# Two sequence passes, one mean and one buffer of a three-stage kernel are moved across the seam between its first two stages

## What is computed

```
X   = fft(fft(x, axis=1), axis=2).real          # a spectrum: [2, 3008, 256]
xn  = x / sqrt(mean(x*x) + 1e-6) * rms_g        # per token
h   = silu(xn @ w_gate) * (xn @ w_val)          # up to 1536
x2  = h @ w_out                                 # down to 256
h2  = x2 @ w_in                                 # up to 2048
out = (h2 * cos(h2)) @ w_out2                   # down to 256
```

## Time and profile before

| what | value |
|---|---|
| median of three runs | 984.6 us |
| the profiled execution | 984.3 us |
| its span, first to last instruction | 982.5 us |
| TensorE busy | 972.3 us, 99% of the span |
| VectorE busy | 742.9 us |
| ScalarE busy | 638.7 us |
| GpSimd busy | 350.4 us |
| granted TensorE clock | full in all of 40 slices |

### The profile page before, as it was taken

One profiled execution on the slowest core, in us unless ns is written; L12 is line 12 of the kernel. 1 busy time (PEld: TensorE's weight loads), 2 busy tenths in 40 slices (PEclk: granted clock), 3 DMA queues, 4 the chain that ended last, 5 costly groups with the idle time before them and its releaser, 6 DMA issues.

```text
span 982.5 us, 13009 instructions
## 1 busy us (share of the span) xinstructions
PE 972.3 (99%) x4518; PEld 807.9 (82%) x4518; DVE 742.9 (76%) x1028; ACT 638.7 (65%) x803; POOL 350.4 (36%) x292
## 2 busy tenths in 40 slices
PE   8999999999999999999999999999999999999998
PEld 8978788888888888888888888888888888888886
DVE  6887987768876768877667877767887767887665
ACT  5586778764468774458775448776448776437777
POOL 0377874027730007750007751005661004770000
PEclk9999999999999999999999999999999999999999
DMA  9788002001010001010001010001000000000001
GB/s 332 235 221 235 1 1 53 0 1 43 1 43 1 1 0 42 0 40 2 0 0 42 0 32 11 0 0 42 0 32 0 0 0 7 36 0 0 0 0 42
DMA packets 14082, 36.80 MB, mean 37 GB/s; under 512 B 2618, under 2 KB 6682, under 8 KB 13658
## 3 DMA queue, kind: packets, MB, share of 16 engines
q1 hardware_dynamic: 11978, 31.63, 9.4%
q0 software_dynamic: 2064, 4.72, 2.7%
HBM read 22.35 MB, written 9.26 MB: 32 GB/s over the span
## 4 chain that ended last, share of the span: by engine, by line
PE 91%; DMA 3%; POOL 2%; DVE 2%; issue 1%; ACT 1%; SPq 0%; DVEq 0%; ACTq 0%; POOLq 0%
PE ps L541 30%; PE ps L543 30%; PE ps L542 30%; DMA x_sb<-x 1%; POOL work L1184 1%; PE ps L492 1%; DMA stat<-mean_row 1%; DMA w_lo<-w_f 1%; PE ps L510 1%; PE ps L508 0%; SPq L319 0%; POOL squares L1122 0%; POOL uv_t L1141 0%; POOL w_lo L1104 0%; POOL h_lo L1095 0%
## 5 line engine op out<-in xcount | busy, mean ns | idle before, releaser
L541 PE MATMUL ps<-h_hi,wo_hi 128*128 128x502 f32 x672 | 261.5, 389 | 0.6 <-DVE h_lo L980 0.6
L543 PE MATMUL ps<-h_hi,wo_lo 128*128 128x502 f32 x672 | 261.3, 389 | 0.0
L542 PE MATMUL ps<-h_lo,wo_hi 128*128 128x502 f32 x672 | 261.1, 389 | 0.0
L1095 POOL TENSOR_TENSOR h_lo<-work,h_hi 128x502 fp32r<-128x502 f32 x92 | 101.5, 1111 | 373.8 <-ACT h_hi L782 369.9
L767 ACT ACTIVATE h_hi<-work 128x502 fp32r<-128x502 f32 x132 | 82.4, 626 | 174.2 <-POOL work L1184 173.9
L1082 DVE SCALAR_TENSOR_TENSOR work<-work,ps 128x1004 f32<-128x1004 f32 (+1 forms) x109 | 117.2, 1075 | 95.6 <-ACT work L864 95.2
L1068 DVE SCALAR_TENSOR_TENSOR work<-work,ps 128x1004 f32<-128x1004 f32 (+1 forms) x109 | 116.5, 1074 | 48.0 <-ACT work L850 47.9
L541 PE MATMUL ps<-x_hi,win_hi 128*128 128x502 f32 x384 | 150.0, 391 | 0.0
L541 PEld LDWEIGHTS ps<-h_hi,wo_hi 128*128 128x128 f32 x672 | 126.2, 188 | 28.2 <-issue 0.8
L542 PE MATMUL ps<-x_lo,win_hi 128*128 128x502 f32 x384 | 149.3, 389 | 0.0
L543 PE MATMUL ps<-x_hi,win_lo 128*128 128x502 f32 x384 | 149.2, 389 | 0.0
(11 more groups left out here) (89 smaller groups left out, 1275.7 us busy)
## 6 DMA issues: line engine op xcount, KB each, us to landing
out<-y_sb SPq DMA_DIRECT2D x10, 502.0 KB, 3.0
x_sb<-x SPq DMA_DIRECT2D x6, 768.0 KB, 10.3
w_lo<-w_f POOLq DMA_DIRECT2D x6, 512.0 KB, 7.0
uv_t<-uv_dram SPq DMA_DIRECT2D x6, 502.0 KB, 3.5
wo_raw<-wo SPq DMA_DIRECT2D x1, 2048.0 KB, 8.5
win_raw<-win SPq DMA_DIRECT2D x1, 2048.0 KB, 9.4
raw_b<-w1b SPq DMA_DIRECT2D x3, 512.0 KB, 12.4
raw_a<-w1a SPq DMA_DIRECT2D x3, 512.0 KB, 12.3
```

Of the source, the lines that this page charges most:

```text
L541: nc.tensor.matmul(acc, w_hi, v_hi, start=start, stop=False)
L542: nc.tensor.matmul(acc, w_hi, v_lo, start=False, stop=False)
L543: return nc.tensor.matmul(acc, w_lo, v_hi, start=False, stop=stop)
L1095: nc.gpsimd.tensor_tensor(dst, src, hi.bitcast(F32), ALU.subtract).then_inc(s, 1)
```

## The change

Four things are changed. (1) The last group of three columns becomes one of two and one of a single column; in both DVE takes the second half and its turn, and the turns count on a semaphore of their own, `n1_turned`. (2) `plus[1]` moves out of `pq` to an address 1024 bytes into `x2_hi`, a buffer that is written and read only in the second half of a tile, when `plus` is not in use. (3) `sequence(32)` and `sequence(33)` move behind item 1's two up products and the eighth mean, which itself moves behind the second half of item 1; on ACT the last `uv_copy` and `mean_copy(7)` stand behind item 0's silu, ahead of `square(8)`; the seventh mean is taken at step 33 and not at step 32. (4) `w1_add(2)` is issued two places sooner on GpSimd.

```diff
-        plus = [sb(f"plus{i}", [N], o_pq + i * TB // 2) for i in range(2)]
+        plus = [sb("plus0", [N], o_pq), sb("plus1", [N], o_x2 + 1024)]
...
-        GROUPS = [range(i, i + 3) for i in range(0, H // 2, 3)]
+        GROUPS = [range(i, i + 3) for i in range(0, H // 2 - 3, 3)] + [range(H // 2 - 3, H // 2 - 1), range(H // 2 - 1, H // 2)]
...
-            return (1, 0) if g == NG - 1 else (0, 1)
+            return (1, 0) if g >= NG - 2 else (0, 1)
...
-        RMS_AT = [8, 9, 15, 20, 24, 28, 32]
+        RMS_AT = [8, 9, 15, 20, 24, 28, 33]
...
-            pe.wait_ge(n1_out, 3 * NG)
+            pe.wait_ge(n1_out, 3 * NG - 4)
+            pe.wait_ge(n1_turned, 4)
...
                 up1(t, 1, halves=(0,))
-                if first:
-                    rms(RMS_LATE[0])
-                else:
+                if not first:
                     down(t - 1, ITEMS - 1, tokens=(0,))
                 up1(t, 1, halves=(1,))
                 if not first:
                     down(t - 1, ITEMS - 1, tokens=(1,))
+                if first:
+                    rms(RMS_LATE[0])
+                    sequence(LAST - 2)
+                    sequence(LAST - 1)
...
             up1(0, 0, halves=(0,))
-            sequence(LAST - 2)
-            sequence(LAST - 1)
+            pe.wait_ge(pq_out, LAST)
             pe.wait_ge(mean_out, len(RMS_AT))
...
-                for c in range(1 if g == NG - 1 else 2):
+                for c in range(1 if g >= NG - 2 else 2):
...
-            for p in range(LAST // 2):
+            for p in range(LAST // 2 - 1):
...
                     if first and i == 0:
+                        uv_copy(LAST // 2 - 1)
+                        mean_copy(RMS_LATE[0])
                         square(MEANS - 1)
-                        mean_copy(RMS_LATE[0])
...
-            dve.wait_ge(n1_done, 2 * NG - 1)
-            ms = GROUPS[-1]
...
+            for g in (NG - 2, NG - 1):
+                ms, bank = GROUPS[g], (2 * g + 1) % 4
+                dve.wait_ge(n1_done, 2 * g + 1)
...
             w1_add(1)
+            w1_add(2)
             add_squares(5)
             scale_uv(0)
             scale_u128(0)
-            w1_add(2)
             add_squares(6)
```

More of the change, by code:

```diff
@@ L154, in build @@
         zeros = sb("zeros", [P], o_pq)
-        plus = [sb(f"plus{i}", [N], o_pq + i * TB // 2) for i in range(2)]
+        plus = [sb("plus0", [N], o_pq), sb("plus1", [N], o_x2 + 1024)]
+        assert o_work + 4 * GCOLS <= o_x2 + 1024 and o_x2 + 1024 + 4 * N <= o_hid - UVB
         o_end = o_pq + pad(max(TB, 16 * DIM))
@@ L180, in build @@
         raw_a_in, raw_b_in = ([sem(f"raw_{ab}_in{i}") for i in range(3)] for ab in "ab")
-        even_done, odd_done, folded, n1_done, n1_main, n1_last, n1_out, seq1_turned = (sem(n) for n in (
-            "even_done", "odd_done", "folded", "n1_done", "n1_main", "n1_last", "n1_out", "seq1_turned"))
+        even_done, odd_done, folded, n1_done, n1_main, n1_last, n1_turned, n1_out, seq1_turned = (sem(n) for n in (
+            "even_done", "odd_done", "folded", "n1_done", "n1_main", "n1_last", "n1_turned", "n1_out", "seq1_turned"))
         pq_done, pq_out, uv_done, uv_main = (sem(n) for n in ("pq_done", "pq_out", "uv_done", "uv_main"))
@@ L903, in _ @@
             nc.vector.tensor_scalar(w128[:, :], sm[:, 3:], g128, None, ALU.mult).then_inc(g_done, 1)
-            dve.wait_ge(n1_done, 2 * NG - 1)
-            ms = GROUPS[-1]
[L906 to L916, removed]
+            for g in (NG - 2, NG - 1):
+                ms, bank = GROUPS[g], (2 * g + 1) % 4
+                dve.wait_ge(n1_done, 2 * g + 1)
+                nc.vector.tensor_copy(
+                    g_sb[:, :, 1, :, 2 * ms[0]:2 * ms[-1] + 2],
+                    ps[:, bank, 0:len(ms) * COLS1].rearrange("p (n b k) -> p b k n", b=BATCH, k=2 * K1)
+                    ).then_inc(n1_last, 1)
+                dve.wait_ge(n1_last, g - NG + 3)
+                for part in range(2):
+                    nc.vector.tensor_scalar(
+                        g_sb[0:1, :, 1, part::2, 2 * ms[0]:2 * ms[-1] + 2],
+                        ps[0:1, bank, 1 - part:len(ms) * COLS1:2].rearrange(
+                            "p (n b k) -> p b k n", b=BATCH, k=K1),
+                        1.0 if part else -1.0, None, ALU.mult).then_inc(n1_turned, 1)
             dve.wait_ge(g_done, 3)
```

## The result

In 21 executions the changed kernel took a median of 987.93 us (984.23 to 991.87), and the kernel before, on the same chip, 984.83 us (983.80 to 988.08). The ratio is 1.0032, with a 95% interval of 1.0019 to 1.0044. The forecast was 985.8, in a range of 983.9 to 987.1, so the loss is more than twice the forecast's, and lies outside the range.

A forecast was written before the change was run, and what follows sets the result against it. TensorE's last wait, at 109.81 us, set by a side chain through GpSimd and the DMA queues, was taken to bound the kernel. It moves by +1.2: 984.6 + 1.2 = 985.8 us, range 983.9 to 987.1.

The forecast's parts named there:

- the part up to the first tile: Before tile 0: w1_add(2) fits GpSimd's idle time until 50.37; tile 0 starts at 58.45, 0.73 us sooner, up to 1.1.
- Rival C: w1_add(2)'s new place fails, delaying add_squares(5), tile 0's scaling, then DVE; decides past 50.37 by over 0.73: 986.9 us, chance 0.13.
- The seam: Items 0 and 1 of tile 0: ACT's rounding waits behind moved copy and squares; GpSimd's product ends at 74.0, +1.3 us.
- The queues: DMA behind the seam: wo2 and uv stores go 1.6 us later; the sixth weight transfer lands 1.2 us later.
- Part 1: At the start, the cut last group: 0.1 us won, between 0.4 lost and 0.5 won, worth nothing to the end.
- Part 2: The new address of plus[1]: costs 0 by itself, at most 5 us of DVE time beside a never idle TensorE.
- A: TensorE's lead lasts: the sixth transfer starts 0.73 to 1.1 us sooner, ACT's copy not holding item 1: 983.7 us, chance 0.12.
- B: The delay is swallowed in the sixth transfer's landing, 1 to 2 us of which may be luck: 984.6 us, chance 0.20.
- D: plus[1]'s address or the new order disturbs TensorE's rhythm in all tiles: 0.2%, 1.7 us, to 986.5 or more, chance 0.03.
- the side chain: GpSimd, the sixth transfer, win2's load and the last mean's spread set TensorE's last wait at 109.81, and so the end.

The follow-up runs named there:

- e1: The kernel before with only the third weight transfer, w1_add(2), issued ahead of add_squares(5): 986.75 us, ratio 1.0013.
- e2: The changed kernel with only w1_add(2) put back behind the scaling: 986.32 us, ratio 1.0013.
- e4: The changed kernel with DVE's tenth weight mixing one step sooner, at step 25 and not 26: 985.91 us, ratio 1.0009.
- e0: The changed kernel itself measured again, beside the others on one chip: 989.21 us in 12 runs, ratio 1.0039.
- e9: The kernel before with w1_add(2) sooner, seventh mean at step 33 and tenth mixing at step 25; seam and groups left: 983.42 us, ratio 0.9993.
- e11: The changed kernel with the tenth mixing at step 25 and the last mean's spread sent ahead of the win2 load: 983.57 us, ratio 0.9994.
- e10: The kernel before with only the last mean's spread sent ahead of the six transfer waits and the win2 load: 983.50 us, ratio 0.9990.
- e7: The kernel before with only the last group of columns cut in two and one: 984.86 us, ratio 1.0006.
- e3: The kernel before with plus[1] moved and the seam's new order (passes, eighth mean, last copy), seventh mean still at step 32: 986.72 us, ratio 1.0017.
- e12: The kernel before with w1_add(2) sooner, seventh mean at 33, tenth mixing at 25, last spread ahead of win2; seam and groups left: 983.03 us, ratio 0.9982.

## Why the prediction was wrong

**The failed step.** It is the sentence "49.05 + 1.19 = 50.24 just fits", in the part up to the first tile, with its silence on DVE. By the records the issue did not fit. It starts 0.30 us after ACT's row has ended, which the sum left out: in the changed kernel ACT ends at 50.37 and the issue starts at 50.67. The kernel before had shown the same 0.30 at its next transfer, where ACT ends at 62.01 (GpSimd, 60 to 74):

```profile
62.31 1.21 POOL L1104 DMA_DIRECT2D w_lo<-w_f  x1 [3.12 <-ACT w_lo L720]
```

So the issue ran from 23.48 to 24.67 us behind `features`, past the 24.50 at which the squares were due. Their record still starts at 24.50 in both kernels (50.37 - 25.87 and 51.69 - 27.19), but ends at 25.55 and not at 25.34. The mixing starts at 25.22 and the scaling at 25.31 or 25.32 in both; so the race was there before, and most likely those 0.21 us turned it, though no run moved them alone. Whoever wins takes all: DVE waits for four GpSimd instructions, 3.6 us more than its 0.74. I had looked for the cost on GpSimd (its issue, its squares, its scaling) and not on the engine it shares with. That the issue's new place starts the fault is shown: `e1` makes it with that edit alone, `e2` takes it away by undoing it, and `e4` by moving the other party.

**Rival C** named the right place and the right edit, with a chance of 0.13, but the wrong victim. It even had the condition, an issue that comes later than in the sum, but let it count only past 0.73 us, and the issue ended 0.17 us past the squares' place. It had the scaling late. The scaling came on time; it was DVE that was late. Its price of 1.6 + 0.7 = 2.3 us came nearest to the median of all that were given (986.9 against 987.93), by another way, and that is luck.

**Why the size was missed even so.** TensorE's idle time of 2.2 us brings the clock down in some executions, up to 3.0 us more. Nothing in the prediction asked what an idle time near 57 would do to the clock. And the outcome differs between executions of one program: `e1` and `e0` show two sets, with a gap of 1.2 and of 1.4 us between them. A margin of 0.13 us (50.24 against 50.37) in a sum of rows is less than the 0.30 us that it left out, and should have widened the range upward.

**The part up to the first tile, otherwise right.** Where DVE wins, tile 0 comes 0.89 us sooner behind `features` than before (`e4`; `e9` 0.84), where 0.73 was forecast and 1.1 the bound. Of the 1.26 us of wait ahead of the seventh mean at most 0.36 us (`e2`) is left in any profile with that mean at step 33.

**The seam.** Mechanism right, size in parts. From tile 0's start to the end of product 1 the forecast has 74.0 - 58.45 = 15.55 us (its own terms add up to 74.08); it is 15.27 to 15.30 in six profiles with the new seam (`e11` among them), and 13.55 to 13.58 in six with the old one (`e10`, whose clock had fallen, has 14.89). The rest of the step's sum, that GpSimd has "no idle time to give" up to the sixth issue, was wrong by 0.27 us (5.28 against 5.55). The issue came at 78.78 in `e4`, forecast 79.6. The first `down` waits 1.20 us, forecast about 2.

**The queues.** In `e4` the chain of waits (start, us, what) reads:

```profile
78.78 6.96 DMA w_lo<-w_f
...
87.43 9.39 DMA stat<-mean_row
```

The sixth transfer landed at 85.74, and before at 85.66, though issued 0.50 later. The fifth landed 1.29 us later for an issue 0.77 later, near the 1.22 us of the `wo2` load, as the forecast has it for transfers behind that load. But the 0.08 of the sixth doesn't fit it. The load of `win2` and the spread behind it then took longer, the spread 9.39 and not 9.03 us, and landed at 96.82, forecast 97.2. The last wait is 0.81 later, forecast 1.2; the median of `e4` is 1.2 above the kernel before (985.91 against 984.68). So the sum was right within its range, and the way to it only partly; that the two differences nearly cancel is luck. What holds the fifth transfer can be seen from the packets of GpSimd's queue: the first stands at 77.59 before and at 78.84 in `e4`, 1.25 us later, as much as the load ahead of it (1.22) and not as its issue (0.77). What sets the landing of the sixth was not settled.

**Part 1.** 0.1 won was forecast between 0.4 lost and 0.5 won; 0.12 lost is what `e7` shows in its profile. It was priced as worth nothing, and in the median it is.

**Part 2, rivals A, B and D.** From the last wait on all kernels that have one take the same time, to some 0.1 us: the span grew by 4.3 us in the changed kernel, 6.3 in `e0` and 0.8 in `e4`, and the last wait by 4.17, 6.32 and 0.81. So D is out, and `plus[1]` costs nothing there (D's own sum was off too: 984.6 + 1.7 is 986.3, not 986.5). A, that the lead lasts, is refuted by `e3` and `e4`: the sixth issue is never sooner with the new seam. B, that the delay is swallowed, has 0.42 of the sixth transfer's delay on its side, but the last wait still moved.

**That the side chain sets the end** was right, and `e11` shows it from the other side: taking the spread out of that chain takes 1.8 us off `e4`, while `e10` and `e12` have the same sign at 0.65 and 0.8.

**What stays open.** Why DVE's request wins in one execution and loses in the next, and so the mechanism of the race itself, of which only the trigger and the price are shown; why the clock falls after 2.15 us idle in one and not after 2.16 in another; and whether the lower sets of `e1` and `e0` are indeed the executions in which DVE won, since all profiles of these two codes fell in the upper ones.

## What to carry to other kernels

Where a margin between two engines that read the same memory is a few tenths of a microsecond, ask who gets shut out and for how long: count every instruction that follows back to back on the other engine, and not the one alone. Count too the time between one engine's last row and the start of what it releases, here 0.30 us. Measure such a kernel with enough runs to see two sets, since one profile shows only one of them. And before time is won on the main engine, follow the chain that sets its last wait: here the last spread, sent a few lines sooner, took 0.65 to 1.8 us off, while the reordering of TensorE by itself cost 2.0.

## What the runs showed of the hardware

**Shut out by a run, not by one instruction.** A DVE instruction with two inputs in SBUF (128 x 512, 0.74 us alone) took 4.32 or 4.33 us in three profiles (the changed kernel, `e0`, `e1`), and ended 0.56 or 0.57 us after the last of four GpSimd instructions that stood back to back. In every one of the 14 profiles, too, a mixing that took 0.9 us or more ended 0.55 to 0.57 us after the end of a GpSimd instruction. How many it stays out for is not fixed: in the kernel before, the eleventh got in behind one addition of squares (56.84, 1.16 us), and in `e10` it stayed out over two (2.94 us), though each time a transfer's issue stood between them. The other way round the GpSimd instruction waits for one DVE instruction: 3.04 for 2.47, 1.31 for 1.05. The Trainium skill, SBUF — State Buffer, section SBUF: two separate sides, has the ports as an exclusive lock that whoever starts first keeps "for the whole instruction". The trace agrees that it is exclusive; here it was kept over four instructions.

**The clock.** After 2.15 us idle the granted clock stood at 0.50 (1.2 GHz) in the 6 us from 56 to 62 in one execution (`e0`), and after 2.16 us idle at 1.00 in another. Matmuls that stand 0.23 us apart at the full clock stood 0.42 apart in `e10`. The mean clock of the changed kernel's 21 executions was 0.999 or 1.000 in the eight up to 986.34 us, and 0.996 to 0.998 in the nine from 989.26 on; so part of its scatter is the clock.
